# Five token pairs of 512 columns and one of 448, in place of four of 512 and two of 480, in a kernel of an FFT filter and two MLPs

## The chip, the cores and the metric

The kernel runs on one core of one Trainium2 chip. The metric is the device time of one execution in microseconds (us), the median of several runs. Lower is better.

## The reference, cut to what matters

The input has 2 batches of 3008 tokens with 256 features. Each feature's sequence is filtered in the frequency domain, and then all 6016 tokens go through two MLPs of the same shape (256 to 2048 to 256). The first has a leaky ReLU, the second a squared ReLU. Everything is float32.

```
X = rfft(x, axis=1);  y = irfft(X * (filt_r + 1j*filt_i), n=3008, axis=1)
x = y.reshape(6016, 256)
h = x @ w_in;   g = maximum(0.01*h, h);       x = g @ w_out      # first MLP
h = x @ w2_in;  r = maximum(h, 0); g = r*r;   out = g @ w2_out   # second MLP
```

The MLPs treat every token by itself, so it doesn't matter to them where one batch ends and the next begins.

## The kernel before, in words

**Stages.** The FFT part fills the first 115 us or so: small float32 matmuls against tables of sines and cosines (L880 to L935), whose results go through a DRAM scratch buffer. Its last step writes the filtered tokens into YT, a buffer of 128 partitions x 2 halves of the features x 6016 token columns. The batches lie one behind the other in YT: batch 0 has columns 0 to 3007, batch 1 columns 3008 to 6015. From there on the two MLPs run as one long loop, each reading its tokens from YT and writing its results back into YT.

**Token pairs.** The MLP loop takes tokens in pairs of column blocks: two neighbouring blocks of equal width w are the two "halves" of one step of a Strassen-Winograd scheme, which needs 7 block products in place of 8 for x @ w_in. PAIR_W (L17) lists the widths w. Before, each batch is cut into pairs of 512, 512 and 480 (2 x 1504 = 3008 columns), so that there are NP = 6 pairs, with widths 512, 512, 480, 512, 512, 480. The function pair_cols (L174) gives a pair's first column and width, and width (L180) gives the width that belongs to a slot.

**Slots.** For each pair the loop walks over KU = 8 chunks of 256 hidden features. One pair and one chunk is a slot; there are 2 x 6 x 8 = 96 slots, numbered s. In each slot TensorE does 45 matmuls of w columns each: 7 products for x @ w_in (`up`, L970) and 4 units of 2 products each for g @ w_out (`down`, L1030). Each product is three passes, because both operands are split into a high and a low part of type float32r: high by high, high by low, low by high (L966 to L968 and L974 to L976). Each pass has weights of its own, 128 x 128, which are loaded just ahead of it.

**Order on TensorE.** The loop at L1057 interleaves the groups of `up` for slot s with units of `down` that lie LAG = 6 units behind, one slot and a half. So in the first slot and a half of a pair the `down` matmuls still have the width of the pair before.

**The other engines.** ScalarE copies products out of PSUM (snap1, L622, once per slot; snap2, L629; snap7, L637; whole_d, L645) and rounds the activated values (L651). VectorE does the sums of the scheme (L797, L805, L814), the activation (L821 in the first MLP, L823 in the second) and the low parts (L829): 11 operations per slot, each w columns wide. In slot k = 1 of a pair ScalarE also copies out the finished result of the pair before (`evacuate`, L653), and in the first MLP it rounds pieces of the second MLP's weights beside (w2_round, L540, in slots 8 to 39). GpSimd prepares the sums and low parts of the next pair's input (x_forms, x_split).

**End.** SyncE sends each finished pair of the second MLP to DRAM while the next is computed. Of the last pair, L330 to L334 send the parts as they come out of PSUM.

Of the kernel before, what the change touches and what calls it, by code (L numbers as in the profile page):

```python
# [5 lines left out]
B, S, D, F = 2, 3008, 256, 2048  # L6
# [7 lines left out]
TOK = B * S  # L14
FCH = F // 128
HALF = S
PAIR_W = (512, 512, 480)  # L17
NP = B * len(PAIR_W)
KU = FCH // 2
SLOTS = 2 * NP * KU  # L20
XG = (2, 2, 2, 2, 4, 4, 4, 4)
# [7 lines left out]
def fft_mlp_kernel(nc, x, filt, dft, tab, w1i, w1o, w2i, w2o, out):  # L29
# [60 lines left out]
    with ExitStack() as ctx:  # L90
# [83 lines left out]
        def pair_cols(p):  # L174

            q = p % NP
            b, i = q // len(PAIR_W), q % len(PAIR_W)
            return b * S + 2 * sum(PAIR_W[:i]), PAIR_W[i]

        def width(s):  # L180

            return PAIR_W[s // KU % len(PAIR_W)]

        def cols(a, d, t, p):

            c, w = pair_cols(p)
            return a[:, d, c + t * w:c + t * w + w]
# [24 lines left out]
        def _(sp):  # L212
# [96 lines left out]

            last1 = (NP - 1) * KU  # L310
            sp.wait_ge(pw_out, 32 * CHUNKS)
# [9 lines left out]

            for p in range(NP, 2 * NP - 1):
                c, w = pair_cols(p)
                sp.wait_ge(evac[0], p + 1)
                sp.wait_ge(evac[1], p + 1)
                sp.dma_start(out[:, :, c:c + 2 * w], YT[:, :, c:c + 2 * w]).then_inc(out_done, 16)

            c, w = pair_cols(2 * NP - 1)
            sp.wait_ge(evac[0], 2 * NP)
            sp.dma_start(out[:, :, c:c + w], YT[:, :, c:c + w]).then_inc(out_done, 16)  # L330
# [865 lines left out]
```

## Time and profile before

| | |
|---|---|
| median of 3 runs | 1092.52 us (1092.36 to 1093.44) |
| the profiled execution's own time | 1092.61 us |
| its span, first to last instruction | 1090.8 us |
| TensorE matmul busy | 1084.2 us, 99% of the span |
| VectorE busy | 772.2 us, 71% |
| ScalarE busy | 567.8 us, 52% |
| GpSimd busy | 294.8 us, 27% |
| granted TensorE clock | 1.0 of full speed |

"Busy" for matmuls counts from the start of each to its modelled end. Matmuls overlap in the array (each is shown with 0.37 to 0.40 us though a new one starts every 0.21 to 0.23 us), so the busy share doesn't tell how fast the stream of matmuls runs. For that one reads the distance between starts.

### The profile page before, as it was taken

What the parts mean: (1) busy time and instruction counts of PE and PEld (TensorE: products, weight loads), DVE (VectorE), ACT (ScalarE), POOL (GpSimd) and SP (SyncE); (2) the same over time, 40 slices, a digit from 0 to 9 for tenths busy, and PEclk for the clock granted to TensorE, in tenths of its full rate; (3) what the DMA queues carried; (4) which work ended last, traced back from release to release, by engine and by line L of the source; (5) the groups of instructions that cost most, each with busy time, mean ns of one, the idle gap of its engine ahead of it and who ended that gap; (6) DMA issues with size and microseconds to landing.
All of it is one profiled execution on the core that took longest, in us unless ns stands there. A gap on an engine that the chain in (4) does not pass through costs nothing.

```text
span 1090.8 us, 14076 instructions
## 1 busy us (share of the span) xinstructions
PE 1084.2 (99%) x5108; PEld 913.0 (84%) x5108; DVE 772.2 (71%) x1184; ACT 567.8 (52%) x983; POOL 294.8 (27%) x285
## 2 busy tenths in 40 slices
PE   9999999999999999999999999999999999999998
PEld 9888888888888888888888888888888888888887
DVE  2996889777677767767766676676676667667665
ACT  3555655555455555555554554554554554554543
POOL 0789344224333333333220220220210220220000
PEclk9999999999999999999999999999999999999999
DMA  9778400012112212212344200000100000000000
GB/s 321 226 227 260 146 1 1 23 44 59 44 44 59 53 35 59 53 37 52 103 136 134 69 1 1 39 1 1 39 1 1 37 1 1 39 1 1 39 1 37
DMA packets 70053, 66.09 MB, mean 61 GB/s; under 512 B 40800, under 2 KB 55648, under 8 KB 69984
## 3 DMA queue, kind: packets, MB, share of 16 engines
q1 hardware_dynamic: 69408, 64.47, 19.2%
q8 instruction: 41, 0.67, 0.3%
q10 hardware_dynamic: 576, 0.72, 0.2%
q14 instruction: 28, 0.23, 0.1%
HBM read 41.19 MB, written 23.99 MB: 60 GB/s over the span
## 4 chain that ended last, share of the span: by engine, by line
PE 98%; DMA 1%; DVE 1%; ACT 0%; issue 0%; ACTq 0%; DVEq 0%
PE PS L967 16%; PE PS L966 16%; PE PS L968 16%; PE PS L974 14%; PE PS L976 14%; PE PS L975 14%; PE PS L907 3%; PE PS L917 3%; PE PS L880 2%; PE PS L935 1%; PE PS L896 1%; DMA X<-in_x 1%; DVE YL L763 0%; DVE YT L743 0%; DVE XT L781 0%
## 5 line engine op out<-in xcount | busy, mean ns | idle before, releaser
L651 ACT ACTIVATE GH<-GF 128x512 fp32r<-128x512 f32 (+1 forms) x384 | 238.7, 622 | 226.2 <-DVE GF L823 116.3
L829 DVE TENSOR_TENSOR GL<-GF,GH 128x512 fp32r<-128x512 f32 (+1 forms) x384 | 258.8, 680 | 106.0 <-ACT GH L651 99.5
L967 PE MATMUL PS<-GL,WOH 128*128 128x512 f32 (+1 forms) x768 | 296.4, 386 | 0.0
L966 PE MATMUL PS<-GH,WOH 128*128 128x512 f32 (+1 forms) x768 | 296.3, 386 | 0.0
L968 PE MATMUL PS<-GH,WOL 128*128 128x512 f32 (+1 forms) x768 | 296.1, 386 | 0.0
L974 PE MATMUL PS<-XH,WIH 128*128 128x512 f32 (+1 forms) x672 | 260.0, 387 | 0.1
L976 PE MATMUL PS<-XH,WIL 128*128 128x512 f32 (+1 forms) x672 | 259.2, 386 | 0.0
L797 DVE TENSOR_TENSOR GF<-PS,GF 128x512 f32<-128x512 f32 (+1 forms) x96 | 65.3, 680 | 165.6 <-ACT GF L622 165.4
L966 PEld LDWEIGHTS PS<-GH,WOH 128*128 128x128 f32 x768 | 144.2, 188 | 27.7
L967 PEld LDWEIGHTS PS<-GL,WOH 128*128 128x128 f32 x768 | 144.1, 188 | 27.6
L968 PEld LDWEIGHTS PS<-GH,WOL 128*128 128x128 f32 x768 | 144.1, 188 | 27.6
L974 PEld LDWEIGHTS PS<-XH,WIH 128*128 128x128 f32 x672 | 126.1, 188 | 26.2 <-ACT SN L629 1.4
L975 PE MATMUL PS<-YL,WIH 128*128 128x512 f32 (+1 forms) x384 | 148.0, 385 | 0.0
L976 PEld LDWEIGHTS PS<-XH,WIL 128*128 128x128 f32 x672 | 126.1, 188 | 24.1
L622 ACT ACTIVATE GF<-PS 128x512 f32<-128x512 f32 (+1 forms) x96 | 56.6, 590 | 168.5 <-PE PS L968 167.5
L821 DVE SCALAR_TENSOR_TENSOR GF<-GF 128x512 f32<-128x512 f32 (+1 forms) x192 | 142.4, 781 | 1.7
L823 DVE SCALAR_TENSOR_TENSOR GF<-GF 128x512 f32<-128x512 f32 (+1 forms) x192 | 121.7, 674 | 1.7
L975 PE MATMUL PS<-XL,WIH 128*128 128x512 f32 (+1 forms) x288 | 111.1, 386 | 0.0
L422 POOL TENSOR_TENSOR YL<-YT,XH 128x1024 fp32r<-128x1024 f32 (+1 forms) x22 | 52.6, 2392 | 137.5 <-DVE GL L829 137.5
L645 ACT ACTIVATE GF<-PS 128x512 f32<-128x512 f32 (+1 forms) x96 | 56.7, 591 | 57.7 <-PE PS L976 57.7
L975 PEld LDWEIGHTS PS<-YL,WIH 128*128 128x128 f32 x384 | 72.1, 188 | 13.6
L805 DVE TENSOR_TENSOR GF<-PS,GF 128x512 f32<-128x512 f32 (+1 forms) x96 | 64.5, 672 | 0.0
(74 smaller groups left out, 957.7 us busy)
## 6 DMA issues: line engine op xcount, KB each, us to landing
zu<-U SPq DMA_DIRECT2D x32, 192.0 KB, 2.9
V<-zu SPq DMA_DIRECT2D x12, 512.0 KB, 5.0
FL<-in_filt SPq DMA_DIRECT2D x16, 336.0 KB, 4.2
X<-in_x SPq DMA_DIRECT2D x8, 512.0 KB, 10.5
out_y<-YT SPq DMA_DIRECT2D x4, 1024.0 KB, 4.3
wi<-PWH SPq DMA_DIRECT2D x16, 224.0 KB, 2.5
wi<-PWL SPq DMA_DIRECT2D x16, 224.0 KB, 3.1
WIH<-wi SPq DMA_DIRECT2D x8, 448.0 KB, 3.5
```

What stands on the lines that cost most here:

```text
L651: nc.scalar.activation(GH[:, g, 0:width(s)], GF[:, g, 0:width(s)], ACT.Copy).then_inc(g_hi[kind], 1)
L797: nc.vector.tensor_tensor(h, PS[:, YB, 0:w], h, ALU.add).then_inc(h_sb[UA], 1)
L805: nc.vector.tensor_tensor(h, PS[:, XB[s % 2], 0:w], h, ALU.add).then_inc(h_sb[UB], 1)
L821: nc.vector.scalar_tensor_tensor(h, h, 0.01, h, ALU.mult, ALU.max).then_inc(g_sb[kind], 1)
L823: nc.vector.scalar_tensor_tensor(h, h, 0.0, h, ALU.max, ALU.mult).then_inc(g_sb[kind], 1)
L829: nc.vector.tensor_tensor(GL[:, g, 0:w], GF[:, g, 0:w], GH[:, g, 0:w].bitcast(f32), ALU.subtract).then_inc(g_lo[kind], 1)
L966: nc.tensor.matmul(acc, wh, xh, start=first, stop=False)
L967: nc.tensor.matmul(acc, wh, xl, start=False, stop=False)
L968: return nc.tensor.matmul(acc, wl, xh, start=False, stop=last)
L974: nc.tensor.matmul(acc, wh, xh, start=first, stop=False, skip_group_check=not first)
L975: nc.tensor.matmul(acc, wh, lo, start=False, stop=False, skip_group_check=not first)
L976: return nc.tensor.matmul(acc, wl, xh, start=False, stop=True, skip_group_check=not first)
```

## The change

PAIR_W becomes one list for all 6016 tokens, and pair_cols and NP no longer count by batch. The pairs now have widths 512, 512, 512, 512, 512, 448. Their sum is 3008 as before, so each MLP still streams the same number of token columns in the same number of matmuls. The third pair crosses from batch 0 into batch 1 (columns 2048 to 3071). Pairs 0 and 1 are as before, pairs 3 and 4 keep their width and begin 64 columns further on, and pair 5 covers columns 5120 to 6015. `width` needs no edit: it takes the slot's pair modulo the length of PAIR_W, which is now 6.

```
-PAIR_W = (512, 512, 480)
-NP = B * len(PAIR_W)
+PAIR_W = (512, 512, 512, 512, 512, 448)
+NP = len(PAIR_W)
...
         def pair_cols(p):

             q = p % NP
-            b, i = q // len(PAIR_W), q % len(PAIR_W)
-            return b * S + 2 * sum(PAIR_W[:i]), PAIR_W[i]
+            return 2 * sum(PAIR_W[:q]), PAIR_W[q]
```

## Rows read from the trace of the kernel before

**Rows 1.** The page: busy time by engine, and the granted clock in 40 slices.
```profile
PE 1084.2 (99%) x5108; PEld 913.0 (84%) x5108; DVE 772.2 (71%) x1184; ACT 567.8 (52%) x983; POOL 294.8 (27%) x285
...
PEclk9999999999999999999999999999999999999999
```

**Rows 2.** The page: the chain that ended last, shares by engine and line.
```profile
PE 98%; DMA 1%; DVE 1%; ACT 0%; issue 0%; ACTq 0%; DVEq 0%
PE PS L967 16%; PE PS L966 16%; PE PS L968 16%; PE PS L974 14%; PE PS L976 14%; PE PS L975 14%; PE PS L907 3%; PE PS L917 3%; PE PS L880 2%; PE PS L935 1%; PE PS L896 1%; DMA X<-in_x 1%; DVE YL L763 0%; DVE YT L743 0%; DVE XT L781 0%
```

**Rows 3.** Groups by line and form: busy us, mean ns | idle before.
```profile
L966 PE MATMUL PS<-GH,WOH 128*128 128x512 f32 x512 | 199.3, 389 | 0.0
...
L829 DVE TENSOR_TENSOR GL<-GF,GH 128x512 fp32r<-128x512 f32 x256 | 175.1, 691 | 69.9 <-ACT GH L651 66.1
...
L966 PEld LDWEIGHTS PS<-GH,WOH 128*128 128x128 f32 x768 | 144.2, 188 | 27.7
...
L821 DVE SCALAR_TENSOR_TENSOR GF<-GF 128x512 f32<-128x512 f32 x128 | 100.9, 827 | 1.1
...
L966 PE MATMUL PS<-GH,WOH 128*128 128x480 f32 x256 | 97.0, 379 | 0.0
...
L530 ACT ACTIVATE YT<-PS 128x448 f32<-128x448 f32 x2 | 1.1, 540 | 0.6 <-PE PS L935 0.6
```

**Rows 4.** Timeline of TensorE, width 512: start us, us; first and last of twelve.
```profile
199.79 0.39 PE L967 MATMUL PS<-GL,WOH 128*128 128x512 f32 x1
...
202.28 0.39 PE L974 MATMUL PS<-XH,WIH 128*128 128x512 f32 x1
```

**Rows 5.** Timeline of TensorE and its weight loads (PEld), width 480: start us, us.
```profile
300.58 0.38 PE L967 MATMUL PS<-GL,WOH 128*128 128x480 f32 x1
...
300.80 0.39 PE L968 MATMUL PS<-GH,WOL 128*128 128x480 f32 x1
300.81 0.19 PEld L966 LDWEIGHTS PS<-GH,WOH 128*128 128x128 f32 x1
301.03 0.37 PE L966 MATMUL PS<-GH,WOH 128*128 128x480 f32 x1
...
301.24 0.38 PE L967 MATMUL PS<-GL,WOH 128*128 128x480 f32 x1
```

**Rows 6.** Timeline of ScalarE, L622 alone: slots 10 and 15, width 512.
```profile
215.52 0.60 ACT L622 ACTIVATE GF<-PS 128x512 f32<-128x512 f32 x1 [0.97 <-PE PS L968]
...
266.52 0.60 ACT L622 ACTIVATE GF<-PS 128x512 f32<-128x512 f32 x1 [2.02 <-PE PS L968]
```

**Rows 7.** The same, slots 42 and 47, width 480.
```profile
538.53 0.57 ACT L622 ACTIVATE GF<-PS 128x480 f32<-128x480 f32 x1 [1.34 <-PE PS L968]
...
587.36 0.57 ACT L622 ACTIVATE GF<-PS 128x480 f32<-128x480 f32 x1 [1.95 <-PE PS L968]
```

**Rows 8.** The same, first MLP: slots 25, 26, 33 and 34.
```profile
365.35 0.60 ACT L622 ACTIVATE GF<-PS 128x512 f32<-128x512 f32 x1 [1.94 <-PE PS L968]
375.77 0.60 ACT L622 ACTIVATE GF<-PS 128x512 f32<-128x512 f32 x1 [0.97 <-PE PS L968]
...
447.17 0.60 ACT L622 ACTIVATE GF<-PS 128x512 f32<-128x512 f32 x1 [2.02 <-PE PS L968]
457.45 0.60 ACT L622 ACTIVATE GF<-PS 128x512 f32<-128x512 f32 x1 [0.98 <-PE PS L968]
```

**Rows 9.** The same, second MLP: slots 63 and 74, either side of pair 8.
```profile
749.91 0.60 ACT L622 ACTIVATE GF<-PS 128x512 f32<-128x512 f32 x1 [2.02 <-PE PS L968]
...
858.77 0.60 ACT L622 ACTIVATE GF<-PS 128x512 f32<-128x512 f32 x1 [1.30 <-PE PS L968]
```

**Rows 10.** Waits of the weight loads, 130 us to the end: total, times, longest.
```profile
PEld PS L974 <- ACT SN L629: 1.0, 4, 0.4
```

**Rows 11.** Chain that ended last, in order: start us, us; a float32 stream.
```profile
100.50 11.63 PE PS L935 x104
```

**Rows 12.** Timeline of ScalarE at the end: last copy out of PSUM.
```profile
1086.50 0.57 ACT L707 ACTIVATE YT<-PS 128x480 f32<-128x480 f32 x1 [0.33 <-PE PS L968]
```

## The prediction

> **What bounds the kernel now.** I read the page's busy shares first: matmuls are busy 99% of the span and the granted clock is at its upper level, 2.4 GHz, in every slice [rows 1]. The chain that ended last agrees: 98% of it is TensorE, and the six passes of the MLP products make up 90% of it [rows 2]. So only what changes the pace of the matmul stream, or stops it, can move the time. The groups by form say that nothing stops it at either width: idle before the passes is 0.0 [rows 3], and the waits of the weight loads after 130 us come to 1.0 us in 4 places [rows 10]. The other engines have room. VectorE does 11 operations of about 0.69 us per slot of width 512 (the four of L821 take 0.83 in the first MLP), so 8.1 us out of a slot of 10.2, and ScalarE has less.
>
> What is left is the pace itself, and for that I read the timeline. A slot always has 45 matmuls, and the copy at L622 comes once per slot, so the distance between two of them is a slot's time.
> - Width 512: slots 10 to 15 take 51.00 us for 5 slots, 10.200 us each, 226.7 ns per matmul [rows 6]. The single starts are even: 11 distances in 2.49 us, 226 each [rows 4].
> - Width 480: slots 42 to 47 take 48.83 us for 5 slots, 9.766 us each, 217.0 ns per matmul [rows 7]. Here the starts are uneven: the distances are 0.22, 0.23 and 0.21 us [rows 5].
>
> At 2.4 GHz and one column per cycle, 512 columns are 213.3 ns and 480 are 200.0. So a matmul costs 13.3 ns beyond its columns at 512, but 17.0 ns at 480. The step from 512 to 480 takes 32 columns away, worth 13.3 ns, and gives back 9.7. This is where the case is decided, since the change alters neither the number of matmuls nor the sum of their columns: 4 x 512 + 2 x 480 = 5 x 512 + 448 = 3008, with 360 matmuls per pair in each MLP (8 slots of 45). If the cost of a matmul is a straight line in its width, the change is worth nothing. If something at 480 already keeps a matmul from being as fast as its columns, then 448 gets less than a straight line gives, and the change loses.
>
> **The change part by part.**
>
> *Pairs 2 and 8 go from 480 to 512.* Both widths are in the trace, so this term is safe. In the second MLP, slots 63 to 74 span the 480 pair with its transitions: 858.77 - 749.91 = 108.86 us for 11 slots [rows 9]. Eleven slots at 512 are 112.20. That adds 3.34. In the first MLP the same stretch, slots 15 to 26, runs from 266.52 to 375.77, 109.25 us [rows 6, 8]. It holds a stall: slot 25 takes 10.42 us [rows 8], where ScalarE has the copy-out of the pair before and a rounding of second-MLP weights ahead of snap2, for which TensorE waits (0.4 us is the longest such wait) [rows 10]. Between two 512 pairs the same slot of the next pair takes 10.28 [rows 8], 0.08 more than a plain one. I take that for the two slots k = 1 in the stretch: 112.20 + 0.16 = 112.36, which adds 3.11. Together +6.45 us. By the plain difference it would be 16 slots x 0.434 = 6.9; the rest is transitions that the 480 pair now has and no longer will, and the stall. I keep 6.3 to 6.9 as its bounds.
>
> *Pairs 5 and 11 go from 480 to 448.* No pass of this kind with 448 columns is in the trace, so this term has to be bounded. Nearest rows: 217.0 ns at 480 and 226.7 at 512.
> - Upper end: 448 costs what 480 costs, 217.0 ns. Fewer columns won't take longer, and the other engines' operations shrink with the width (L622 takes 0.60 us at 512 and 0.57 at 480) [rows 6, 7]. The term is 0.
> - Straight line through the two widths: 9.7 ns less, 207.3 ns, slot 9.33 us; 16 slots x 0.434 = -6.9 us.
> - Columns only: 13.3 ns less than 480, 203.7 ns; 720 matmuls x 13.3 = -9.6 us. With the 13.3 ns beyond its columns that 512 has, 200.0 ns; -12.3 us. That is the lower end.
>
> I take the upper end, 0. The reason is the kind of difference between the widths. At 512 every start is 226 or 227 ns after the last: one process sets the pace, the columns plus 32 cycles. At 480 some starts come after 0.21 us, which is just 480 plus 32 cycles (213.3 ns), and others after 0.22 or 0.23 to make up for it, while the slot keeps to 9.766. Matmuls that could run at 213 are held by a second process of about 217 ns per load and matmul. A pace that was already fixed when the width fell to 480 has no reason to fall at 448. Each pass has a weight load of its own of 188 ns [rows 3], which starts when the matmul before starts [rows 5], so a process per load that doesn't know the width is at hand. Against it: in the FFT part the same shape of load, with plain float32 data, goes every 112 ns (11.63 us for 104) [rows 11], so a load as such isn't bound to 217. If the second process depends on the width a little, the cost lies between the upper end and the straight line; above that line it can't be a minimum of two, below it can. So as long as the larger of two growing costs sets the pace, this change can't be faster.
>
> *Pair 2 crosses the batches.* YT is one row of columns, the input forms of pair 2 are made in slots 9 to 14, and all of YT is written before pair 1's forms begin. Instruction counts stay. Cost 0, hidden by GpSimd at 27%. If it weren't, the first matmul of the pair would wait; no wait of that kind is in the trace.
>
> *Reload of weights between the MLPs, stores.* The reload follows the last 448 pair at the pace of its slots, and each chunk has 8 slots until it is needed; cost 0. *Tail:* the last copy out of PSUM at L707 takes 0.57 us [rows 12], and a 448-wide copy 0.54 [rows 3]: -0.03.
>
> **Sum.** 6.45 + 0 - 0.03 = +6.4 us. On the profiled execution, span 1090.8 and 1.8 around it: 1092.6 + 6.4 = 1099.0; it lies 0.1 above the median of 1092.52, so 1098.9.
>
> **The rivals.**
> - *A straight line in the width.* 448 costs 207.3 ns. Then -6.9 against +6.4: -0.5, 1092.0. For it: two points always lie on a line, and a load can go faster [rows 11]. Against it: the uneven starts at 480 only, which a single process wouldn't have.
> - *In between.* The second process shrinks with the width, but less than the line, say 212 ns: 720 x (212 - 217) = -3.6, so +2.8, 1095.3.
> - *The pace comes loose below 480 (the other side).* The 17 ns beyond the columns at 480 is a mishap of how that width falls into step with the loads, and 448 runs at columns plus 13.3 to 17 ns, 200.0 to 203.7: 1092.5 + 6.4 - 9.6 = 1089.3, down to 1086.6. It decides in favour of the change as soon as a 448 matmul costs less than 208.1 ns (217.0 - 6.4 / 0.720). For it: starts at 0.21 us show that the array can take a matmul so soon. Against it: slots of 480 all keep to the same 9.77 us, in both MLPs, and never come loose.
>
> The Trainium skill, "TensorE: Matmul & The Clock Gate", section "Back-to-back issue gap", gives N / 2.4 + 2.5 ns for an isolated warm matmul, which is a line in the width and speaks against any change. By it 512, 480 and 448 columns are estimated at 215.8, 202.5 and 189.2 ns and the change at 0. The trace has 226.7 and 217.0 and another slope. The same section says that in a stream of loads and matmuls both set the spacing, which is the form of my forecast; it has no figure for this kind of data.
>
> **How the numbers follow.** Forecast (floor at 217) 0.58; in between 0.14; line 0.17; loose 0.11. A measurement of this kernel can tell 0.2%, 2.2 us, from no change. The floor is slower, and so is most of the case in between (448 over 211 ns, 0.11 of its 0.14): slower 0.69. The line and the rest of the case in between are within 0.2%: 0.20. Loose gives faster: 0.11. The range reaches down to the line with 1 us of slack, 1091.0, and up to 1099.9 (the 6.9 for the first term and 0.6 for stalls that new transitions may bring). It leaves out the loose case and a little above.
>
> **What would show it.** In the changed kernel slots 17 to 23 have to take 10.20 us each. In the last pair of each MLP (slots 42 to 47 and 90 to 95) the distance of the copies at L622 decides: 9.77 us is the floor, 9.33 the line, 9.17 or less loose. Matmuls of 448 should start 217 ns apart on average, still unevenly. The stall of slot 25 should shrink from 0.2 us or so to under 0.1. The prediction is wrong if the 448 slots fall under 9.6 us, or if TensorE waits for another engine at the new widths.

## The result, and the profile after

The changed kernel takes 1089.64 us (median of 10 runs, 1089.14 to 1091.89) against 1092.93 us for the kernel before (10 runs as well). The ratio is 0.9971, with a 95% interval of 0.9962 to 0.9980. It is 3.3 us faster, where 6.4 us slower was forecast. The profiled execution took 1089.14 us with a span of 1087.4 us, 3.4 less than before. The line numbers after are one lower from L178 on (L622 is now L621); the three down passes, L966 to L968, are now L965 to L967.

The page shows the same picture as before, busy shares and chain included; TensorE's clock is again at 2.4 GHz in every slice [rows 1, 2]:

```profile
PE 1081.5 (99%) x5108; PEld 914.0 (84%) x5108; DVE 771.8 (71%) x1184; ACT 567.5 (52%) x983; POOL 294.9 (27%) x285
...
PEclk9999999999999999999999999999999999999999
...
PE 98%; DMA 1%; DVE 1%; ACT 0%; issue 0%; ACTq 0%; DVEq 0%
```

The three stretches that decide it are read from the once-per-slot copy, L621 after. First the second MLP, slots 63 and 74, as in [rows 9]:

```profile
748.31 0.60 ACT L621 ACTIVATE GF<-PS 128x512 f32<-128x512 f32 x1 [2.02 <-PE PS L967]
...
860.51 0.60 ACT L621 ACTIVATE GF<-PS 128x512 f32<-128x512 f32 x1 [1.31 <-PE PS L967]
```

These are 112.20 us in place of 108.86, the +3.34 of the prediction to the last digit. Then slot 25, from its copy to that of slot 26, which stands for slots 9 and 17 too [rows 8]:

```profile
368.94 0.60 ACT L621 ACTIVATE GF<-PS 128x512 f32<-128x512 f32 x1 [2.02 <-PE PS L967]
379.34 0.60 ACT L621 ACTIVATE GF<-PS 128x512 f32<-128x512 f32 x1 [0.98 <-PE PS L967]
```

This slot takes 10.40 us by these rows (10.41 in slots 9 and 17), 0.2 more than a plain one. Last, the 448 pair of the first MLP, slots 43 and 47 (the group that answers to [rows 7]):

```profile
550.32 0.54 ACT L621 ACTIVATE GF<-PS 128x448 f32<-128x448 f32 x1 [1.64 <-PE PS L967]
...
586.80 0.54 ACT L621 ACTIVATE GF<-PS 128x448 f32<-128x448 f32 x1 [1.77 <-PE PS L967]
```

Four slots in 36.48 us are 9.120 us each, 202.7 ns per matmul. At 480 it was 217.0 [rows 7]. Single starts on TensorE's timeline at 448 columns (to compare with [rows 5]):

```profile
1080.07 0.36 PE L966 MATMUL PS<-GL,WOH 128*128 128x448 f32 x1
1080.27 0.36 PE L967 MATMUL PS<-GH,WOL 128*128 128x448 f32 x1
1080.47 0.37 PE L965 MATMUL PS<-GH,WOH 128*128 128x448 f32 x1
1080.67 0.36 PE L966 MATMUL PS<-GL,WOH 128*128 128x448 f32 x1
```

Set side by side in the two profiled executions, from the copies of equal slots: pair 2 with its transitions (slots 15 to 26) +3.36, pair 8 (63 to 74) +3.34, pair 5 (39 to 50) -5.09, pair 11 to the last copy out (87 to the end) -5.14, everything else +0.1 (slot 9, of a pair of 512 before and after, is +0.15 of it). The sum is -3.4 us, the whole difference of the spans.

### The profile page after: what moved, and what is told of

Read it like the earlier page. It is cut to its first block, busy times and chain, and to the rows that moved or that the text cites. A ratio compares the mean times of both kernels' runs of the same rounds, so it can differ in the third digit from the quotient of the medians.

```text
span 1087.4 us, 14076 instructions
## 1 busy us (share of the span) xinstructions
PE 1081.5 (99%) x5108; PEld 914.0 (84%) x5108; DVE 771.8 (71%) x1184; ACT 567.5 (52%) x983; POOL 294.9 (27%) x285
## 4 chain that ended last, share of the span: by engine, by line
PE 98%; DMA 1%; DVE 1%; ACT 0%; issue 0%; ACTq 0%; DVEq 0%
PE PS L967 16%; PE PS L966 16%; PE PS L965 16%; PE PS L973 14%; PE PS L975 14%; PE PS L974 14%; PE PS L906 3%; PE PS L916 3%; PE PS L879 2%; PE PS L934 1%; PE PS L895 1%; DMA X<-in_x 1%; DVE YL L762 0%; DVE YT L742 0%; DVE XT L780 0%
## 5 line engine op out<-in xcount | busy, mean ns | idle before, releaser
L828 DVE TENSOR_TENSOR GL<-GF,GH 128x512 fp32r<-128x512 f32 (+1 forms) x384 | 258.6, 680 | 105.2 <-ACT GH L650 99.3
L967 PE MATMUL PS<-GH,WOL 128*128 128x512 f32 (+1 forms) x768 | 295.8, 385 | 0.0
L965 PE MATMUL PS<-GH,WOH 128*128 128x512 f32 (+1 forms) x768 | 295.8, 385 | 0.0
L966 PE MATMUL PS<-GL,WOH 128*128 128x512 f32 (+1 forms) x768 | 295.8, 385 | 0.0
L966 PEld LDWEIGHTS PS<-GL,WOH 128*128 128x128 f32 x768 | 144.2, 188 | 26.9
L965 PEld LDWEIGHTS PS<-GH,WOH 128*128 128x128 f32 x768 | 144.2, 188 | 26.9
L967 PEld LDWEIGHTS PS<-GH,WOL 128*128 128x128 f32 x768 | 144.2, 188 | 26.8
L621 ACT ACTIVATE GF<-PS 128x512 f32<-128x512 f32 (+1 forms) x96 | 56.5, 588 | 167.0 <-PE PS L967 166.0
L820 DVE SCALAR_TENSOR_TENSOR GF<-GF 128x512 f32<-128x512 f32 (+1 forms) x192 | 142.2, 780 | 1.7
```

Source lines behind the costliest of these rows:

```text
L820: nc.vector.scalar_tensor_tensor(h, h, 0.01, h, ALU.mult, ALU.max).then_inc(g_sb[kind], 1)
L828: nc.vector.tensor_tensor(GL[:, g, 0:w], GF[:, g, 0:w], GH[:, g, 0:w].bitcast(f32), ALU.subtract).then_inc(g_lo[kind], 1)
L965: nc.tensor.matmul(acc, wh, xh, start=first, stop=False)
L966: nc.tensor.matmul(acc, wh, xl, start=False, stop=False)
L967: return nc.tensor.matmul(acc, wl, xh, start=False, stop=last)
```

## The experiments

**1. The stream alone, by width.** The first question was whether the three costs (226.7 ns at 512, 217.0 at 480, 202.7 at 448) are TensorE's own, or come from the other engines or from where operands lie in this kernel. The kernel leaves out the whole reference and has this stream for each width w, with three matmuls to an accumulation group (matmuls that add up in one accumulator) and six accumulators in turn (cut to what matters, m is 128 and off is 0):

```
for i in range(60):
    nc.tensor.matmul(PS[0:m, (i // 3) % 6, 0:w], WR[:, i % 8, 0:m], XR[:, off:off + w], start=i % 3 == 0, stop=i % 3 == 2)
```

> No part of the reference is computed: one stream of float32r matmuls with 128x128 weights, three to an accumulation group, nothing else running, 60 in a row at each width: 512 to 440 in steps of 8, then 432, 424, 416, 400, 384, 368, 352, 320, 288, 256, 192, 128 and 512 again. The changed kernel's slots give 226.7 ns at 512, 217.0 at 480 and 202.7 at 448, that is 32, 41 and 38 cycles beyond the columns. Theory A (the pace is TensorE's own and depends on the width's divisibility by 64 or 32): the stream repeats the three values within 1 ns, and the widths that are multiples of 64 (512, 448, 384, 320, 256) have fewer cycles beyond their columns than the widths between them. Theory B (TensorE's own, a floor under which the load can't go, at about 217, which is not hit by every width): 472 and 464 stay at 217 and 456 or 448 fall. Theory C (480 is slowed in the kernel by the other engines or by where its operands lie): alone, 480 takes 213.3 ns (480 + 32 cycles), and every width has the same 32 cycles down to where the loads (112 ns) bound it.

Busy time by stretch, TensorE, stream alone. Each stretch is as long as it is from the first start at one width to the first start at the next, laid 0.05 us later, and holds 60 starts (the two more that it counts began before it). The widths are 512, 504, 496, 488, 480, 472, 464, 456, 448, 440, 400, 320, 256 and 192 in this order:

```profile
30.85:44.45 13.60, 13.60 (x62) 1.00 0.00 0
44.45:58.05 13.60, 13.60 (x62) 1.00 0.01 1
58.05:71.45 13.40, 13.40 (x62) 1.00 0.00 0
71.45:84.65 13.20, 13.20 (x62) 1.00 0.00 0
84.65:97.65 13.00, 13.00 (x62) 1.00 0.00 1
97.65:110.45 12.80, 12.80 (x62) 1.00 0.00 0
110.45:122.98 12.53, 12.53 (x62) 1.00 0.01 1
122.98:135.50 12.52, 12.52 (x62) 1.00 0.00 0
135.50:147.66 12.16, 12.16 (x62) 1.00 0.01 1
147.66:159.66 12.00, 12.00 (x62) 1.00 0.00 0
194.30:205.10 10.80, 10.80 (x62) 1.00 0.00 0
235.19:243.99 8.80, 8.80 (x62) 1.00 0.00 0
251.89:259.08 7.19, 7.19 (x62) 1.00 0.00 0
259.08:265.76 6.68, 6.68 (x62) 1.00 0.00 0
```

A stretch over 60 is the time of a matmul; at 2.4 GHz, less the columns, it gives the cycles beyond them:

| columns | 512 | 504 | 496 | 488 | 480 | 472 | 464 | 456 | 448 | 440 | 400 | 320 | 256 | 192 |
|---|---|---|---|---|---|---|---|---|---|---|---|---|---|---|
| ns | 226.7 | 226.7 | 223.3 | 220.0 | 216.7 | 213.3 | 208.8 | 208.7 | 202.7 | 200.0 | 180.0 | 146.7 | 119.8 | 111.3 |
| cycles beyond | 32 | 40 | 40 | 40 | 40 | 40 | 37 | 45 | 38 | 40 | 32 | 32 | 32 | 75 |

The stream alone repeats all three values (512 settles at 226.7), so theory C is out for them: no other engine has a part in it. (At 504, 488 and 456 columns the kernel and the stream alone do differ, see experiments 4 and 5.) Theory B, the floor of the prediction, is out as well: there is no step at 217, and the stream goes on down to 111 ns. There it has a floor, 111.3 ns at 192 columns and 111.2 at 128. That this is the pace of the weight loads fits the 112 ns of [rows 11], but no run varies the load at these widths. Theory A holds for 512, 320 and 256, but 448 has 38 and 400, which isn't a multiple of 64, has 32. The rule by divisibility therefore isn't the rule. What stands is a cost of columns plus 32 to 45 cycles in this table (28 at 288 columns, 131.7 ns), with no order that I can name, and 512 no dearer than 504. The prediction's sign of a second process, uneven starts, isn't one either: at 488 columns, with 40 cycles beyond, the single starts come evenly every 220 ns. The same 480 columns start 215 to 218 ns apart in this kernel and 212 and 221 in turn in the next one, with the same mean of 216.7.

**2. Which term carries the cycles.** The same stream with fewer weight columns (m), another start column (off), and with every matmul a group of its own.

> No part of the reference is computed: the same stream alone, 60 matmuls each at 512, 480 and 448 columns with weights of 128, then 96, 64 and 32 columns; then 128 again with the moving operand beginning 16 and 32 columns further on; then 480 and 448 with every matmul a group of its own. If the cycles beyond the columns belong to the weight load, they shrink with the weights' columns: at 512 from 32 to about 8 with 32-column weights, and the odd value at 480 vanishes. If they belong to the moving operand's reading, weights of 32 columns cost what weights of 128 do, and an offset of 16 or 32 columns changes 480. If they belong to the accumulation, the last two differ from the first.

Busy time by stretch, the second kernel: 448 columns with 128 weight columns, then 512, 480 and 448 with 32 weight columns.

```profile
57.48:69.64 12.16, 12.16 (x62) 1.00 0.00 0
147.65:161.55 13.90, 13.90 (x62) 1.00 0.00 0
161.55:174.36 12.81, 12.81 (x62) 1.00 0.00 1
174.36:186.49 12.13, 12.13 (x62) 1.00 0.00 0
```

With a quarter of the weights, 512 costs 231.7 ns, more than with all of them; 480 falls to 213.5 and 448 stays at 202.2. So the cycles don't belong to the size of the load, though they change with it. Start columns change them too (512 from column 32: 232.2 ns), and so does the grouping (448 with single groups: 206.5). None of the three single causes stands; each moves the value, to between 32 and 48 cycles beyond the columns.

**3. Order and crossing alone.** One row over both batches, with the widths of before.

```
-PAIR_W = (512, 512, 512, 512, 512, 448)
+PAIR_W = (512, 512, 512, 512, 480, 480)
```

> The changed kernel with widths 512, 512, 512, 512, 480, 480: one row over both batches, a pair that crosses them, but the widths of the kernel before. If only the widths count, as I think, it takes the time of the kernel before within 0.5 us (1092.5), since four of the eight transitions between the widths go (up to -0.3) and stalls of 0.2 us in the first slots of pairs 1 to 3 stand as in the changed kernel. If crossing the batches or the order is what made the changed kernel faster, it takes about 1089.6.

It takes 1092.24 us, a ratio of 0.9998 (0.9989 to 1.0008) to the kernel before. Crossing the batches and the order are worth nothing that can be measured; the gain is in the widths.

**4. and 5. Other widths with the same sum.** If the table above is the cost, other lists of six widths with the sum 3008 have to come out where it says, also on the slow side.

```
+PAIR_W = (504, 504, 504, 504, 504, 488)      # fourth
+PAIR_W = (512, 512, 512, 512, 504, 456)      # fifth
```

> Whole kernel, widths 504 five times and 488: the same 3008 columns in the same number of matmuls, and no pair narrower than 488. If the pace of each width is the one that the stream alone had (504: 226.7 ns, 488: 220.0, 512: 226.7, 480: 217.0 in the kernel), each MLP takes 360 matmuls of each width: 5 x 226.7 + 220.0 = 1353.3 against 4 x 226.7 + 2 x 217.0 = 1340.8 of the kernel before, times 0.72: +9.0 us, 1101.7. A straight line in the width, or any cost by columns alone, says 0 and 1092.6.

> Whole kernel, widths 512 four times, 504 and 456: eight columns of the changed kernel's last pair moved to the fifth. By the stream alone 504 costs as much as 512 (226.7) and 456 costs 208.7 against 202.7 at 448: 6.0 ns x 720 = +4.3 us over the changed kernel, 1093.9, which is slower than the kernel before. By columns alone: 0, 1089.6.

The fourth takes 1106.28 us, ratio 1.0124 (1.0108 to 1.0139); the fifth 1093.09 us, ratio 1.0006 (0.9997 to 1.0015). A cost by columns alone is refuted for good: moving eight columns from each of the 512 pairs to the last cost 16.6 us against the changed kernel. The rank is right, the fourth's size is not: +13.7 where +9.0 was expected. The fifth is 3.5 us over the changed kernel where 4.3 was expected; that it is slower than the kernel before is not shown, since its interval holds 1. ScalarE's timeline says more, slots at 488 columns (two slots) and, from the fifth kernel, at 456 (three slots):

```profile
1063.97 0.58 ACT L621 ACTIVATE GF<-PS 128x488 f32<-128x488 f32 x1 [2.04 <-PE PS L967]
...
1084.08 0.58 ACT L621 ACTIVATE GF<-PS 128x488 f32<-128x488 f32 x1 [2.04 <-PE PS L967]
```

```profile
1043.61 0.55 ACT L621 ACTIVATE GF<-PS 128x456 f32<-128x456 f32 x1 [1.85 <-PE PS L967]
...
1071.59 0.55 ACT L621 ACTIVATE GF<-PS 128x456 f32<-128x456 f32 x1 [1.85 <-PE PS L967]
```

A 488 slot takes 10.055 us, 223.4 ns per matmul where the stream alone had 220.0; a 504 slot takes 10.23, 227.4 against 226.7; a 456 slot 9.327, 207.3 against 208.7. So at these three widths the real stream adds 0.7 or 3.4 ns or takes 1.4 away, while 512, 480 and 448 repeat the stream alone within 0.3 ns. Which of its differences (tiles, start columns, order of the groups) does it isn't shown. The 504 and 488 pairs account for some 5 us of the fourth kernel (0.7 ns x 3600 matmuls and 3.4 x 720), about the part that was missing.

**6. The 448 pair first.**

```
+PAIR_W = (448, 512, 512, 512, 512, 512)
```

> Whole kernel, the 448 pair ahead of the five of 512 in place of behind them. The passes cost the same. The chain of single steps in which ScalarE and VectorE prepare the first pair (112 to 120 us) gets 12% shorter operations, about 8 of 0.6 to 0.7 us: -0.6, against +0.1 at the end where the last copy and transfer are 512 wide: 1089.1. Rival: in slots 0 to 7 the weights are prepared as the slots go (GpSimd and ScalarE), and slots of 9.1 in place of 10.2 us outrun them; then TensorE waits in these slots and it is slower than 1089.6.

It takes 1090.94 us, ratio 0.9985 (0.9976 to 0.9995), 1.3 us slower than the changed kernel. The two intervals overlap, but the waits that the rival foretold are in the trace (weight loads, 115 to 200 us):

```profile
PEld PS L965 <- DVE GL L828: 2.1, 3, 0.8
PEld PS L973 <- ACT SN L628: 0.4, 1, 0.4
PEld PS L973 <- DVE YL L762: 0.2, 1, 0.2
```

The longest of them are for VectorE's low parts (L828). Slots 3, 4 and 5 take 9.68, 9.77 and 9.76 us in place of 9.12. In slots 4 and 5 VectorE's three activations (L820) take 4.71 us together while GpSimd prepares weights and the next pair's input; they took nearly as long, 4.68, in slot 5 of the changed kernel, which lost nothing by it over slots 5 and 6 together (20.41 us against 20.40). The narrow pair is better placed at the end, where no weights are prepared beside it.

**7. and 8. The stall in slot k = 1.** In the changed kernel TensorE's weight loads wait for snap2 in three places, 130 us to the end, as much in total as the four of [rows 10]:

```profile
PEld PS L973 <- ACT SN L628: 1.0, 3, 0.3
```

ScalarE's timeline in slot 9 of the changed kernel shows snap2 (L628) right behind the 1.0 us copy-out (L657):

```profile
209.02 1.01 ACT L657 ACTIVATE YT<-PS 128x1024 f32<-128x1024 f32 x1
209.92 0.58 ACT L628 ACTIVATE SN<-PS 128x512 f32<-128x512 f32 x1
```

```
-                if k == 1 and p >= 1:
-                    evacuate(p - 1, 1)
                 if 1 <= s < SLOTS:
                     snap2(s)
+                if k == 1 and p >= 1:
+                    evacuate(p - 1, 1)
```

> The changed kernel with one reordering on ScalarE: in slot k = 1 of a pair snap2 comes ahead of the second copy-out of the pair before, which takes 1.0 us. In the changed kernel slots 9, 17 and 25 take 10.407 us against 10.200, and TensorE waits there for snap2. If that copy-out is what holds snap2, the three slots fall to 10.2 and 0.6 us go: 1089.0. Rival: the copy-out, now 0.6 us later, holds the first matmul of the other half of the accumulators (unit B of the new pair), and as much is lost there: 1089.6 or more, in the second MLP too.

It takes 1088.53 us, ratio 0.9961 (0.9947 to 0.9975). Slots 9, 17 and 25 are now 10.20, and no wait of a weight load is left after 130 us. The three stalls were held by the copy-out as expected, and the accumulators came free in time.

The copy-out always stands ahead of snap2, though, and there is no stall in the second MLP, nor in slot 33 of the changed kernel. What decides it is when the copy-out can begin: ScalarE first rounds an activated value, and VectorE's activation comes late where GpSimd is at a low part of the second MLP's weights (PWL). Slot 9 before, slot 9 after, and slot 33 after:

```profile
206.53 1.16 POOL L388 TENSOR_TENSOR PWL<-PWF,PWH 128x448 fp32r<-128x448 f32 x1
207.17 2.28 DVE L821 SCALAR_TENSOR_TENSOR GF<-GF 128x512 f32<-128x512 f32 x3
...
206.73 1.16 POOL L387 TENSOR_TENSOR PWL<-PWF,PWH 128x448 fp32r<-128x448 f32 x1
207.23 2.42 DVE L820 SCALAR_TENSOR_TENSOR GF<-GF 128x512 f32<-128x512 f32 x3
...
451.88 1.16 POOL L387 TENSOR_TENSOR PWL<-PWF,PWH 128x448 fp32r<-128x448 f32 x1
452.65 2.13 DVE L820 SCALAR_TENSOR_TENSOR GF<-GF 128x512 f32<-128x512 f32 x3
```

The first of the three activations takes 1.07, 1.22 and 0.93 us, and each time ends 0.55 us after GpSimd's operation; in slots 57, 65 and 73, without such a piece, it takes 0.68. The same holds for all 20 of the changed kernel's activations in slots 3 to 34 that take over 0.85 us (L820, up to 2.89): each ends 0.55 or 0.56 us after a GpSimd operation does. GpSimd is later or earlier because it first makes the sums for the next pair, at that pair's width. So the stall goes by the width of the next pair: slot 9 takes 10.26 us with 480 to come (before) and 10.41 with 512 (after), slot 33 takes 10.28 with 480 and 10.20 with 448, and slot 25 of experiment 3, with 480 to come, 10.26. Why VectorE is held no run tests.

The median of this run is 1.1 us under the changed kernel's, though, where the slots account for 0.6. So it ran again beside the changed kernel on one chip:

> The changed kernel again, on the same chip as the two that follow, so that the three can be set side by side: 1089.6.

> The changed kernel with snap2 ahead of the second copy-out in slot k = 1. Three stalls of 0.2 us are gone from the slots: 0.6 us under the changed kernel on the same chip. If it is 1.1 under it as in the run before, half of that is not in the slots and has to be at the start or the end.

1089.69 us (ratio 0.9968, 0.9956 to 0.9979) and 1088.34 us (0.9963, 0.9950 to 0.9975). The intervals overlap, so the times alone don't show a gain; the slots do. From slot 8 on, the two profiles differ by 0.6 us, and from the last slot's copy to the end by nothing (19.4 us in both). The rest lies ahead of slot 8: slot 0 begins at 118.01 us in the one and at 116.76 in the other, and anywhere from 115.5 to 118.0 in the profiles of the changed kernel and its variants with pair 0 at 512 columns. What moves it stays open.

**9. Is it the data type?** The stream alone, now over start columns and kinds of data.

> No part of the reference is computed: one stream of matmuls alone with 128x128 weights, three to a group. First float32r, 448 columns, with the moving operand beginning at column 0, 8, 16, 24, 32, 48, 64 and 80 of its tile; then 512 and 480 at column 64; then bfloat16 at 512, 504, 480, 448 and 256; then plain float32 at 256, 240 and 224 (each matmul is two records). The stream alone had 486.4 cycles for 448 columns from column 0, 480.0 from column 16 and 489.6 from column 32. If the start of the operand decides through its place within 64 columns (256 bytes), column 64 repeats column 0, and column 80 repeats column 16. If the cycles beyond the columns are float32r's own, bfloat16 shows a small constant (2 to 6 cycles) at every width, and so does float32 over its 2 cycles per column.

Busy time by stretch, 60 starts each: float32r at 448 columns from column 0, 8, 16 and 64; then bfloat16 at 512, 480 and 448 (the stretch at 504 is left out).

```profile
33.48:45.65 12.17, 12.17 (x62) 1.00 0.00 0
45.65:58.05 12.40, 12.40 (x62) 1.00 0.00 1
58.05:70.05 12.00, 12.00 (x62) 1.00 0.00 0
106.73:119.12 12.39, 12.39 (x62) 1.00 0.01 1
157.77:170.73 12.96, 12.96 (x62) 1.00 0.01 1
183.48:195.63 12.15, 12.15 (x62) 1.00 0.00 1
195.63:206.98 11.35, 11.35 (x62) 1.00 0.00 0
```

bfloat16 takes 216.0 (it settles at 215.8), 202.5 and 189.2 ns: 6 cycles beyond the columns at each width, evenly, with the same 128 x 128 loads. Plain float32 takes the same 216, 202.5 and 189.2 ns per record at 256, 240 and 224 columns (2 cycles per column). So the 32 to 45 cycles and their uneven course come with float32r. The guess that the place within 64 columns decides is refuted: from column 64 a 448 matmul takes 206.5 ns, from column 0 202.8. From column 16 it takes 200.0, and from column 80 it did so too.

**10. and 11. A start column put to use.** In the 448 pairs the input and ring tiles have 64 columns to spare, so the operands can begin at column 16. This comes on top of the order of experiment 7.

```
+SHIFT = 16
...
+        def span(w):
+
+            o = SHIFT if w == 448 else 0
+            return slice(o, o + w)
...
-                acc, wh, wl, xh = PS[:, bank, 0:w], WIH[:, k, form, :], WIL[:, k, form, :], XH[x][:, hi, 0:w]
+                acc, wh, wl, xh = PS[:, bank, 0:w], WIH[:, k, form, :], WIL[:, k, form, :], XH[x][:, hi, span(w)]
...        (and so in every use of XH, XL, XT, GH, GL and GF in the slots, and where their pairs are prepared)
```

> The changed kernel with snap2 ahead of the copy-out (1088.5) and, in the 448 pairs, the moving operands in the ring and input tiles (41 of 45 matmuls of a slot) begun 16 columns further on. In the stream alone this took a 448 matmul from 202.7 to 200.0 ns. If it carries over, the slots of the 448 pairs fall from 9.120 to 9.01 us and 16 x 0.11 = 1.7 us go: 1086.8. Rival: what matters is how operand, weights and accumulators lie to each other in the stream, and not the start alone, and the slots come out between 9.0 and 9.3: no gain or up to 2 us lost.

> The same with the moving operands of the 448 pairs begun 16 columns further on: slots of 9.03 in place of 9.12 us, 16 of them, 1.4 us under the one with snap2 alone. If start columns don't carry over from run to run, no difference.

It takes 1087.24 us (ratio 0.9953, 0.9937 to 0.9970), and again, beside the two above, 1087.12 us (0.9949, 0.9937 to 0.9962). The copies of slots 43 and 47 (L627 in this kernel):

```profile
549.44 0.55 ACT L627 ACTIVATE GF<-PS 128x448 f32<-128x448 f32 x1 [1.19 <-PE PS L973]
...
585.57 0.55 ACT L627 ACTIVATE GF<-PS 128x448 f32<-128x448 f32 x1 [1.70 <-PE PS L973]
```

Four slots in 36.13 us, 9.033 each: 200.7 ns per matmul, most of what the stream alone had promised (200.0). The expectation of the second run put the 16 slots at 1.4 us. The medians differ by 1088.34 - 1087.12 = 1.2, with intervals that overlap; from slot 0 to the end the two profiles differ by 1.3, since in the first slot and a half of each pair the `down` matmuls are still those of 512 columns. This is the fastest version run, 5.8 us under the kernel before on the same chip (1092.88).

## Why the prediction was wrong, step by step

- *What bounds the kernel:* right. TensorE's stream sets the time, and the widths alone decide (experiment 3).
- *Pairs 2 and 8 to 512:* +6.45 forecast, 3.36 + 3.34 = +6.70 measured. The stall in slots k = 1 was sized at 0.08 and came out at 0.21, twice (slots 17 and 25), which is the +0.25. It was read from slot 33, the pair before one of 480, and put down to a rounding of weights ahead of snap2, of which ScalarE's timeline has none there. The stall goes by the width of the next pair (experiment 7), so slot 25 didn't shrink as forecast: 10.42 before, 10.40 after. The rest is exact, since both widths were in the trace.
- *Pairs 5 and 11 to 448:* 0 forecast, -5.09 and -5.14 measured, -10.2. This is the step that failed. It took the fact that 480 costs more beyond its columns than 512 (41 cycles against 32), together with its uneven starts, for a floor of 217 ns: "A pace that was already fixed when the width fell to 480 has no reason to fall at 448". The runs show no floor there. In the stream alone 488, 480 and 472 columns differ by a full 3.3 ns per 8 columns, the pace of the columns themselves. What looked like a bend between 512 and 480 is 512 being cheap: 504 costs as much as 512. And the uneven starts aren't a sign of a second process (experiment 1).
- *"As long as the larger of two growing costs sets the pace, this change can't be faster":* true as a sentence, but the cost is no such maximum. It isn't even a smooth function of the width. 448 at 202.7 ns lies under the straight line's 207.3.
- *The rivals:* the loose case (0.11) happened. Its price, 200.0 to 203.7 ns, holds the measured 202.7, and its break-even at 208.1 was the right yardstick. Its reason was only half right: 480, with 40 cycles beyond its columns, is no mishap, since six of the nine widths from 440 to 504 have as many; 512, with 32, is the exception. The range left it out; its upper part, 1089.3, is next to the result.
- *Two rows against the floor were at hand and weighed too lightly:* the float32 stream with the same load at 112 ns [rows 11], and starts only 0.21 us apart at 480 [rows 5].
- *Tail and crossing:* right, -0.03 and 0.

The Trainium skill, "TensorE: Matmul & The Clock Gate", section "Back-to-back issue gap", gives N / 2.4 + 2.5 ns for an isolated warm matmul. The stream alone, though it has a load ahead of each matmul, agrees with it for bfloat16, 215.8, 202.5 and 189.2 ns at 512, 480 and 448. For float32r this case measures 226.7, 216.7 and 202.7, and there the measurement decides.

Open is what in float32r makes the cycles beyond the columns go from 32 to 45 and more with width, start column, weight columns and grouping. The runs rule out the size of the load, divisibility by 64 of the width and the place within 64 columns as the single cause, and for 512, 480 and 448 the other engines.

## What to carry to other kernels

Where TensorE's stream is the bound and the data is float32r, measure the time per matmul of each candidate width in a bare stream before choosing how to cut the columns; equal sums of columns are not equal times (16.6 us lay between 504 x 5 + 488 and 512 x 5 + 448). Two widths in a trace don't give the course of a cost, and a bend between two points may be one cheap point. Try the start column of the moving operand too: starting 16 columns further on was worth over 1 us at no cost.

## What the runs showed of the hardware that was not expected

- float32r with a load per matmul takes 32 to 45 cycles more than its columns at 2.4 GHz in the table of experiment 1, down to 256 columns (28 at 288; bfloat16 and float32: 6); at 192 and 128 columns it has a floor of 111 ns.
- 512 and 504 columns cost the same in float32r, 226.7 ns; 464 and 456 nearly so, 208.8 and 208.7.
- At 448 columns the start column alone moves the time from 200.0 ns (column 16) over 202.8 (0) to 206.7 (8).
- While GpSimd ran a 1.16 us operation, VectorE's activation, 0.68 us otherwise, took 0.93 to 1.22 us and ended 0.55 us after it; beside one of 2.85 us it took 2.89 (experiment 7).
